# Values of the local heads kept by tokens, a new order of all steps, and three absolute values on GpSimd in a four-batch attention and mixing kernel

## What is computed

```python
# 1: attention; heads 0-3 see the last 32 keys, heads 4-7 every 32nd key
scores = scale * np.matmul(q, k.transpose(0, 1, 3, 2))
attn = softmax(np.where(masks, scores, -1e9))
x = heads_side_by_side(attn @ v)                  # (4, 576, 512)
# 2: mixing over tokens and channels
theta = x @ w_theta
y = w_tok_r @ (x * np.cos(theta)) + w_tok_i @ (x * np.sin(theta))
u = x + y
x = u + np.maximum(u @ w_ch, 0.0)
# 3: four expert heads with causal attention, weighted by the two largest gate logits
q, k, v = x @ wq[e], x @ wk[e], x @ wv[e]
out += weight_of(e) * (causal_softmax(q @ k.T * scale) @ v @ wo[e])
```

## Time and profile before

| | |
|---|---|
| Median of three runs | 547.89 us (547.35 to 547.92) |
| The profiled execution | 546.84 us |
| Its span in the trace | 545.0 us |
| PE busy | 521.3 us, 96% of the span |
| PE weight loads busy | 451.7 us, 83% |
| DVE busy | 320.3 us, 59% |
| ACT busy | 236.7 us, 43% |
| POOL busy | 109.7 us, 20% |
| Share of PE in the chain that ended last | 79% |

### The profile page before, as it was taken

How to read it: one execution, slowest core, us unless ns; L and a number is a source line. 1 busy time by engine, 2 the same in 40 slices (tenths; PEclk the granted TensorE clock), 3 DMA queues, 4 the chain that set the end, 5 groups by cost and what they waited for, 6 DMA issues and landing times.

```text
span 545.0 us, 13603 instructions
## 1 busy us (share of the span) xinstructions
PE 521.3 (96%) x5577; PEld 451.7 (83%) x5577; DVE 320.3 (59%) x799; ACT 236.7 (43%) x599; POOL 109.7 (20%) x123
## 2 busy tenths in 40 slices
PE   7789999999999999999999999999999999999986
PEld 5567899998966799998877699998986689998764
...
GB/s 217 165 198 38 43 44 183 148 60 33 1 1 20 22 48 127 88 50 46 2 2 1 20 69 79 96 87 34 18 1 1 20 69 1 1 1 1 2 2 87
DMA packets 79997, 28.97 MB, mean 53 GB/s; under 512 B 75200, under 2 KB 75200, under 8 KB 79936
## 3 DMA queue, kind: packets, MB, share of 16 engines
...
## 4 chain that ended last, share of the span: by engine, by line
PE 79%; DVE 8%; SPq 5%; ACT 2%; issue 2%; DMA 1%; POOL 1%; POOLq 0%; DVEq 0%; ACTq 0%
PE acc L1232 41%; PE wide L1232 16%; PE wide L1329 4%; PE turned L1426 3%; PE turned L1367 2%; SPq L606 2%; PE turned L1468 2%; DVE nmax L987 2%; PE wide L1387 2%; PE wide L1308 2%; PE turned L1265 2%; PE turned L1400 1%; PE turned L1353 1%; DMA raw_v<-in_v 1%; SPq L610 1%
## 5 line engine op out<-in xcount | busy, mean ns | idle before, releaser
L772 POOL TENSOR_TENSOR xu_lo<-xt,xu_hi 128x576 fp32r<-128x576 f32 x15 | 21.0, 1414 | 196.4 <-ACT xu_hi L864 196.4
L762 POOL TENSOR_TENSOR probs<-probs,weight 128x128 f32<-128x128 f32 (+4 forms) x36 | 27.0, 769 | 153.6 <-DVE weight L1041 153.6
L842 ACT ACTIVATE probs<-wide,nmax 128x128 f32<-128x128 f32 (+4 forms) x72 | 39.1, 554 | 35.6 <-DVE nmax L987 35.5
L837 ACT ACTIVATE tiled<-wide,nmax 128x64 f32<-128x64 f32 x176 | 39.2, 330 | 22.3 <-DVE nmax L983 17.7
L1232 PE MATMUL wide<-w_tok_hi,z_hi 128*128 128x288 f32 x216 | 47.5, 301 | 0.0
L1232 PE MATMUL wide<-w_tok_lo,z_hi 128*128 128x288 f32 x216 | 46.3, 295 | 0.0
L1232 PE MATMUL wide<-w_tok_hi,z_lo 128*128 128x288 f32 x216 | 46.2, 295 | 0.0
L1232 PE MATMUL acc<-xu_hi,w_ch_hi 128*128 128x288 f32 x128 | 39.2, 306 | 1.0 <-DVE xu_lo L1130 0.9
L853 ACT ACTIVATE pt<-turned 128x384 f32<-128x384 f32 (+1 forms) x32 | 16.5, 516 | 54.3 <-PE turned L1367 54.3
L1232 PE MATMUL acc<-x_hi,w_qk_hi 128*128 128x288 f32 x128 | 39.7, 310 | 0.0
L779 POOL TENSOR_TENSOR z_lo<-absf,z_hi 128x512 fp32r<-128x512 f32 x20 | 26.3, 1317 | 58.4 <-ACT z_hi L901 58.4
...
## 6 DMA issues: line engine op xcount, KB each, us to landing
...
```

Of the source, the lines that this page charges most:

```text
L762: ins = g.tensor_tensor(pr, pr, weight[:, j:j + 1].broadcast_to([P, n]), ALU.mult)
L772: g.tensor_tensor(xu[1][:, p, :], xt[:, p, :], xu[0][:, p, :].bitcast(F32), ALU.subtract)\
L837: e = a.activation(tiled[:, t, hh * W:(hh + 1) * W], wide[slot][:, at0:at0 + W], ACT.Exp, bias=nmax[:, hh, t:t + 1])
L842: e = a.activation(probs[:, hh, to0:to0 + n], wide[slot][:, at0:at0 + n], ACT.Exp, bias=nmax[:, hh, j:j + 1], accum_out=sums[:, hh, j:j + 1])
```

## The change

Three things are changed.

1. The values of the local heads (pairs 0 and 1, channels 0 to 255) are written by `norm` to a new tile `x_loc` for token tiles 0 to 3, instead of to `x_tok`; it lies in the last 1024 columns of the zone of `z`, which is free at that time. Token tile 4 still goes to `x_tok`, so `norm` of a local pair has two multiplications in place of one. `back` transposes from both places. In `products` of batches 1 to 3, tiles 0 to 3, the first 256 channels are now read from `x_loc`, and PE transposes only the last two channel blocks; DVE's two multiplications of 512 columns become four of 256. In batch 0 and for tile 4 everything is as before.
2. The absolute value of theta's tiles 0 to 2 is made by POOL instead of DVE, in two operations: 2·max(f, 0), then less f.
3. All three lists have a new order.

The core of the diff (of the lists one stretch only stands here):

```diff
+ABS_BY_POOL = 3
+
+def absf_of(m):
+    return "absf_pool" if m < ABS_BY_POOL else "absf"
+
+        def x_places(p):
+            cols = tiles(p)[3]
+            if local(p):
+                return [(x_loc[:, :, p, :], 0, NT - 1), (x_tok[:, NT - 1:cols, :], NT - 1, cols)]
+            return [(x_tok[:, 0:cols, :], 0, cols)]
...
 # POOL
+                elif step[0:2] == ("done", "theta") and step[2] < ABS_BY_POOL:
+                    m = step[2]
+                    wait_read(pool, "acc", note[("of",) + step[1:]][0])
+                    f, af = turns[:, m, :], absf[:, m, :]
+                    g.tensor_scalar(af, f, 0.0, 2.0, ALU.max, ALU.mult).then_inc(s["doubled"], 1)
+                    pool.wait_ge(s["doubled"], c.at("doubled", 1))
+                    g.tensor_tensor(af, af, f, ALU.subtract).then_inc(s["absf_pool"], 1)
 # DVE, norm
-                            to = x_tok[:, 0:cols, :].rearrange("p t (h n) -> p h t n", h=2)[:, hs, :, :]
-                            v_.tensor_tensor(to, of[:, :, :, 0:D],
-                                             rec[:, hs, 0:cols].unsqueeze(3).broadcast_to([P, len(range(2)[hs]), cols, D]),
-                                             ALU.mult).then_inc(read[place][u[0]], 1)
+                            for to, lo, hi in x_places(step[2]):
+                                ins = v_.tensor_tensor(to.rearrange("p t (h n) -> p h t n", h=2)[:, hs, :, :],
+                                                       of[:, :, lo:hi, 0:D], rec[:, hs, lo:hi].unsqueeze(3)
+                                                       .broadcast_to([P, len(range(2)[hs]), hi - lo, D]), ALU.mult)
+                            ins.then_inc(read[place][u[0]], 1)
 # DVE, theta
-                    v_.scalar_tensor_tensor(af, f, -1.0, f, ALU.mult, ALU.max).then_inc(s["absf"], 1)
+                    if m >= ABS_BY_POOL:
+                        v_.scalar_tensor_tensor(af, f, -1.0, f, ALU.mult, ALU.max).then_inc(s["absf"], 1)
 # DVE, products
-                    v_.tensor_tensor(absf[0:rows, m, :], x, absf[0:rows, m, :], ALU.mult).then_inc(s["zc"], 1)
+                    if m < NT - 1 and r > 0:
+                        loc = x_loc[:, m, :, :].rearrange("p a n -> p (a n)")
+                        half = DM // 2
+                        v_.tensor_tensor(absf[:, m, 0:half], loc, absf[:, m, 0:half], ALU.mult)
+                        v_.tensor_tensor(absf[:, m, half:DM], x[:, half:DM], absf[:, m, half:DM], ALU.mult)\
+                            .then_inc(s["zc"], 1)
...
 # PE, products
-                    for kc in range(KC):
+                    for kc in range(0 if r == 0 or m == NT - 1 else PAIRS // 2, KC):
...
 # BODY
-    ("max", "s1", 2, 0, 1), ("done", "v", 4), ("copied", "s1", 3, 0), ("exp", "s1", 2, 0, 1), ("values", "s1", 1, 0),
-    ("back", "s1", 0, 0), ("norm", "s1", 1, 0), ("tail", "s1", 3, 0), ("qk", 0, 0), ("back", "s1", 1, 0),
+    ("copied", "s1", 3, 0), ("tail", "s1", 3, 0), ("v", 4), ("qk", 0, 0), ("back", "s1", 0, 0), ("done", "v", 4),
+    ("exp", "s1", 2, 0, 0), ("exp", "s1", 2, 0, 1), ("values", "s1", 1, 0), ("scores", "s1", 3, 0),
```

More of the change, by code:

```diff
@@ L112 @@
-    ("scores", "s1", 3, 0), ("xu", 0), ("xu", 1), ("values", "s1", 2, 0), ("max", "s1", 3, 0, 0),
-    ("warm", 2, "acc", 1), ("warm", 2, "acc", 1), ("max", "s1", 3, 0, 1), ("exp", "s1", 3, 0, 0),
-    ("norm", "s1", 2, 0), ("wtok", 0, "acc"), ("exp", "s1", 3, 0, 1), ("back", "s1", 2, 0),
-    ("done", "wtok", 0, "acc"), ("wtok", 5, "wide"), ("xu", 2), ("turn", "s1", 3, 0), ("wtok", 1, "wide"),
-    ("values", "s1", 3, 0, "turned"), ("norm", "s1", 3, 0, "turned"), ("theta", 0, 0, 3), ("done", "wtok", 5, "wide"),
@@ new lines @@
+    ("tail", "s1", 2, 0, 2), ("piece", 0), ("turn", "s1", 1, 0), ("scores", "s1", 2, 0), ("warm", 1, "acc", 1),
+    ("max", "s1", 2, 0, 0), ("exp", "s1", 2, 0, 0), ("max", "s1", 2, 0, 1), ("values", "s1", 1, 0),
+    ("back", "s1", 0, 0), ("prep", "s1", 3, 0, "acc"), ("copied", "s1", 3, 0), ("norm", "s1", 1, 0),
+    ("exp", "s1", 2, 0, 1), ("tail", "s1", 3, 0, 2), ("xu", 0), ("back", "s1", 1, 0), ("turn", "s1", 2, 0),
+    ("scores", "s1", 3, 0), ("max", "s1", 3, 0, 0), ("xu", 1), ("values", "s1", 2, 0), ("warm", 2, "acc", 1),
@@ new lines @@
+    ("max", "s1", 3, 0, 1), ("warm", 2, "acc", 1), ("norm", "s1", 2, 0), ("piece", 1), ("weights", 2),
+    ("back", "s1", 2, 0), ("exp", "s1", 3, 0, 0), ("exp", "s1", 3, 0, 1), ("turn", "s1", 3, 0), ("wtok", 0, "acc"),
+    ("wtok", 5, "wide"), ("values", "s1", 3, 0, "turned"), ("xu", 2), ("theta", 0, 0, 3), ("done", "wtok", 0, "acc"),
+    ("norm", "s1", 3, 0, "turned"), ("back", "s1", 3, 0), ("theta", 1, 0, 3), ("xu", 3), ("wtok", 1, "wide"),
+    ("theta", 0, 3, 4), ("done", "wtok", 5, "wide"), ("wtok", 6, "wide"), ("theta", 1, 3, 4), ("done", "theta", 0),
@@ L165 @@
-    ("turn", "s3", 1, 1, 0), ("out", 0), ("done", "out", 0), ("scores", "s3", 2, 0), ("max", "s3", 2, 0, 0),
-    ("turn", "s3", 1, 1, 1), ("max", "s3", 2, 0, 1), ("exp", "s3", 2, 0, 0), ("norm", "s3", 2, 0, 0),
-    ("theta", 3, 0, 2), ("theta", 3, 2, 3), ("values", "s3", 1, 1), ("exp", "s3", 2, 0, 1), ("norm", "s3", 2, 0, 1),
-    ("theta", 3, 3, 4), ("trig", 0), ("done", "theta", 3), ("turn", "s3", 2, 0, 0), ("theta", 4, 0, 2),
-    ("products", 0), ("theta", 4, 2, 4), ("turn", "s3", 2, 0, 1), ("done", "theta", 4), ("out", 1),
@@ new lines @@
+    ("theta", 1, 2, 3), ("turn", "s3", 0, 1, 1), ("norm", "s3", 1, 0, 0), ("exp", "s3", 1, 0, 1),
+    ("norm", "s3", 1, 0, 1), ("theta", 1, 3, 4), ("values", "s3", 0, 1), ("scores", "s3", 1, 1), ("done", "theta", 1),
+    ("turn", "s3", 1, 0, 0), ("out", 0), ("max", "s3", 1, 1, 0), ("max", "s3", 1, 1, 1), ("turn", "s3", 1, 0, 1),
+    ("exp", "s3", 1, 1, 0), ("theta", 2, 0, 2), ("theta", 2, 2, 3), ("theta", 2, 3, 4), ("norm", "s3", 1, 1, 0),
+    ("done", "out", 0), ("exp", "s3", 1, 1, 1), ("norm", "s3", 1, 1, 1), ("values", "s3", 1, 0), ("done", "theta", 2),
@@ new lines @@
+    ("scores", "s3", 2, 0), ("theta", 3, 0, 2), ("max", "s3", 2, 0, 0), ("turn", "s3", 1, 1, 0),
+    ("exp", "s3", 2, 0, 0), ("max", "s3", 2, 0, 1), ("turn", "s3", 1, 1, 1), ("theta", 3, 2, 3),
+    ("exp", "s3", 2, 0, 1), ("norm", "s3", 2, 0, 0), ("theta", 3, 3, 4), ("values", "s3", 1, 1), ("theta", 4, 0, 2),
+    ("norm", "s3", 2, 0, 1), ("turn", "s3", 2, 0, 0), ("theta", 4, 2, 4), ("done", "theta", 3), ("trig", 0),
+    ("turn", "s3", 2, 0, 1), ("done", "theta", 4), ("out", 1), ("values", "s3", 2, 0), ("done", "out", 1),
@@ L242, in events @@
     if k == "done":
[L243 removed]
+        return {"out": {f"stored{step[2] % 2}": 16}, "theta": abs_events(step),
                 "wtok": {"wt_hi": 1, "wt_lo": 1}}.get(step[1], {})
```

122 lines of the change are left out of this document (61 added, 61 removed), and 57 rows, old and new, of tables (BODY, EPILOGUE).

## The result

| | before | after |
|---|---|---|
| Median | 547.76 us (547.35 to 547.92, 4 runs) | 542.97 us (541.11 to 543.54, 4 runs) |
| The profiled execution | 546.84 us | 541.11 us |
| Its span | 545.0 us | 539.3 us |

The account below looks back on a forecast made before the run. PE, busy 96%, was taken as the bound, so only its work and idle time count. Savings of 2.2+2.4+0.6+0.7+0.8 = 6.7 us gave 540.1 profiled, 541.2 us as median; the 8-in-10 range was 538.4 to 546.0.

Parts of the forecast that it names:

- transposes left out: Product transposes in the passes: 24 fewer on PE at 0.09 us each, 2.2 us saved, ends 2.1 and 2.6.
- stall at `back` 0: First `back` of each pass: PE's 0.8 us wait before `tail` goes, three times, 2.4 us saved; lower end 0.9.
- the third part: New order in each pass: small waits go, two new ones come, 0.2 us a pass, 0.6 saved; ends 2.4 and -2.1.
- absolute values on GpSimd: 12 pairs of POOL operations, 2.7 us each, hidden behind PE's `theta` and `out` products: no cost.
- order of the prologue: `wtok` 1 fills PE's wait for `xu_lo` 3 at 50.75: 0.7 us saved, ends 0.9 and -0.3.
- order of the epilogue: Three of some ten waits after the passes get work in front: 0.8 us saved, ends 1.2 and -0.7.
- The forecast waits: New waits in a pass at `theta` 0: first block 0.35 us for `xu_lo` 2, last block 0.6 for `xu_lo` 3.
- The rival that GpSimd blocks DVE: POOL's pairs delay DVE up to 2.1 us each, 0.75 of it reaching PE: 9 us, 550.2 us; chance 0.08.
- wave starts wait for `z_lo`: Rival: DVE's four operations ahead of `z_lo` delay wave starts, 1 us each, three times: 544.2 us; chance 0.10.
- some 4: DVE's work over the kernel: net some 4 us less, after losing 12 absolute-value operations and gaining multiplications.
- The rival at 8 chances in 100: Clock falls in the prologue after PE idles 2.9 us before 37.32, costing some 2.8 us: 544.0 us; chance 0.08.

Follow-up runs that it names:

- the kernel with old ends: Prologue and epilogue of the kernel before, passes of the changed one, DVE's absolute values in the first batch: 539.90 us, ratio 0.9835 to the kernel before.
- the changed kernel's second profile: The changed kernel run once more with nothing altered: median 542.91 us, the profiled execution 540.51 us.

## Why the prediction was right, and where it was not

The time lies in the range, and the direction and rough size are right, but the sum was put together from terms that missed on both sides:

| step of the prediction | forecast | measured |
|---|---|---|
| transposes left out | -2.2 | -2.9 (new order), -1.7 (old order) |
| stall at `back` 0 and the third part | -3.0 | -5.5 |
| absolute values on GpSimd | 0 | +1.9 in the prologue, -0.2 in three passes |
| order of the prologue | -0.7 | +0.2 |
| order of the epilogue | -0.8 | +0.2 |

The -0.2 of the absolute values lies within the -5.5. The rest, 0.4 us in the profiled executions, is the varying start of the prologue. That the sum came out near the time is luck: the passes gave 3.2 us more than forecast, the prologue and the epilogue 3.8 us less.

**Transposes.** The step held; 0.09 us each was the price of one in a row of four, and the measured group fell by 0.22, 0.88 to 0.94 us a pass. I had kept to 24 times 0.09 and named 2.6 as the upper end, which is what the group of transposes gives in the new order (1.83 us a pass without `x_loc`, 0.96 with it); the rest of the 2.9, some 0.1 a pass, is spread over the wave's other groups, and no run shows its cause.

**The stall.** It went, and 0.8 is its price (put back, it costs 0.8). But my reason, that `tail` only has to stand elsewhere, was too simple: moved alone it loses 0.3.

**The third part.** This is the term that was mis-sized: 0.2 a pass, where the whole order gave 1.84 a pass (125.91 to 124.07, with the pairs on GpSimd in it), 1.0 more than the stall. The forecast waits came, at four fifths of their size: 0.31 us for `xu_lo` 2 (0.35 forecast) and 0.46 for `xu_lo` 3 (0.6), the latter by the 0.56 us from the masks at 283.50 to `theta`'s last block at 284.06, where 0.10 passed before. What I capped wrongly was the gain: I took the idle time of 1.69 a pass less 0.5 as all there was to win. Overlapping records hid the rest. By groups of matmuls, with the starts of the next group as ends, `turned<-pt,v` fell from 7.23 to 6.58 us a pass, `turned<-ident,probs` from 5.84 to 5.35, `back` from 3.10 to 2.65; the masks ahead of `theta` 0's last block took 0.53 more (1.07 to 1.60), mostly the wait for `xu_lo` 3. And PE's busy time in 123 us is 122.3: only 0.7 idle is left. The 7.1 us that PE is less busy in all show the same.

**Absolute values.** The error that cost time. I priced the pairs where they are hidden, in the passes, and counted 35 us of room there. In the first batch there is no third part between theta and the wave, so POOL's queue goes straight from the pairs to `z_lo`. I had seen that this start is tight, and had put -0.3 in the wrong term. The rival "wave starts wait for `z_lo`" described the event, but at the three passes, by DVE, and 1 us each; there none waits.

**The port.** The rival that GpSimd blocks DVE put DVE's loss at 2.1 us a pair, 25 us for the 12. The pairs cost DVE 3.8 us, 0.3 each, by the kernel with them and the one without. None of that can be seen at PE: the passes are within 0.1 us with and without the pairs. The larger loss, 7.2 us, is that of the multiplications with `x_loc` beside `z_lo`. I had put each of the four multiplications at 0.42, and 3.7 us for all the groups; they cost 10.6 more than the old two. The second multiplications of `norm`, eight of them, cost 1.2; at my bound of 0.46 each they would have been 3.7, and DVE's net gain 1.8 and not "some 4", so that figure did not follow from its own terms. The Trainium skill ("SBUF — State Buffer", section "Who interferes with whom") says that an operation of DVE with both inputs in SBUF contends with GpSimd's reads; the trace agrees, with 0.94 to 1.51 us for a multiplication with `x_loc` that starts while `z_lo` runs, and 0.41 for one from PSUM beside it.

**The clock.** The rival at 8 chances in 100 was the usual case: it fell in five of the six new prologues with the early w_tok load, the first profile alone excepted. It fell in three of the five old ones too (with `x_loc` alone, with `tail` moved, and in the kernel with old ends), so the change is not needed for it. The idle time before it was 1.98 to 4.49 us in the new prologues and 1.65 to 2.23 in the old ones. A fall costs 1.6 us in the changed kernel's second profile and, by the same count, 2.3 to 2.8 in the four variants that were idle for 3.49 us or more; 2.8 were forecast. I cannot say that it makes up the 1.8 us between the profile and the median: the second profiled execution had the fall and took 540.51 us, so how early the values of pair 2 can start counts as much.

**Prologue and epilogue.** `wtok` 1 did fill the wait for `xu_lo` 3 (none is left at that place), but the steps up to it are as much later. In the epilogue the waits moved (8.65 us idle before, 8.70 after). PE's timeline after, the longest two that remain, beside the 0.70 of the earlier trace rows:

```profile
519.20 1.53 PE L1476 MATMUL turned<-pt,v 128*64 128x128 f32 x24 [1.07 <-ACT pt L894]
...
534.39 0.42 PE L1281 MATMUL acc<-w_o_hi,xu_hi 128*64 128x512 f32 x1 [0.77 <-DVE xu_hi L1114]
```

That the waits are a chain of dependent steps with too little independent work left, whatever the order, is my reading; no run tested it.
